# Turning one batch's residual with DMA moves and VectorE transposes, in a Strassen-form MLP kernel

## What is computed

```python
x = decayed_attention(q, k, v, lam)             # laid out as 2 x 768 x 512
h = relu(x^T @ w_tok1) @ w_tok2                 # mixes positions, 768 -> 256 -> 768
u = x + h^T
x = u + relu(u @ w_ch1) @ w_ch2                 # first channel MLP, 512 -> 1536 -> 512
u = x + real(fft2(x))                           # Fourier mixing over positions and channels
un = (u - mean) / sqrt(var + 1e-6)
out = u + relu(un @ w_ch1b) @ w_ch2b            # second channel MLP, 512 -> 2048 -> 512
```

## Time and profile before

| | us |
|---|---|
| median of 3 executions | 566.11 |
| the profiled execution's own time | 565.77 |
| its span, first to last instruction | 563.9 |
| TensorE busy | 559.4 (99%) |
| VectorE busy | 359.0 (64%) |
| GpSimd busy | 256.3 (45%) |
| ScalarE busy | 253.2 (45%) |

### The profile page before, as it was taken

The page is one execution under the profiler, slowest core; times in us unless marked ns, Lnnn a source line. Parts: engine busy times, 40 slices in busy tenths (PEclk is TensorE's granted clock), DMA queues, the critical chain, the costliest instruction groups (busy, mean ns, idle before and its releaser), DMA issues.

```text
span 563.9 us, 9232 instructions
## 1 busy us (share of the span) xinstructions
PE 559.4 (99%) x3412; PEld 499.8 (89%) x3412; DVE 359.0 (64%) x629; ACT 253.2 (45%) x510; POOL 256.3 (45%) x285
## 2 busy tenths in 40 slices
PE   9999999999999999999999999999999999999998
PEld 7889889889989899898988898998989889998996
DVE  5975867766743885467988954679863634344324
ACT  2665335755534444335454443355454433434430
POOL 3663425457534564213767642236563333233301
PEclk9999999999999999999999999999999999999999
DMA  8970303331122121122012220120222212221142
GB/s 324 408 279 3 112 0 118 99 92 52 63 76 74 57 77 60 35 57 74 20 58 75 75 74 20 56 76 20 75 76 75 76 69 63 76 74 57 37 151 112
DMA packets 23726, 48.97 MB, mean 87 GB/s; under 512 B 2170, under 2 KB 3202, under 8 KB 23682
## 3 DMA queue, kind: packets, MB, share of 16 engines
q1 hardware_dynamic: 23088, 46.55, 24.4%
q0 software_dynamic: 448, 1.71, 1.0%
q10 hardware_dynamic: 146, 0.13, 0.1%
HBM read 45.24 MB, written 3.15 MB: 86 GB/s over the span
## 4 chain that ended last, share of the span: by engine, by line
PE 94%; DVE 4%; issue 1%; ACT 0%
PE banks L1200 15%; PE banks L1201 15%; PE banks L1199 15%; PE banks L1479 12%; PE banks L1481 12%; PE banks L1482 12%; PE banks L1272 2%; PE banks L1223 2%; PE banks L1260 2%; PE banks L1316 2%; PE banks L1248 1%; PE banks L1336 1%; PE banks L1211 1%; PE banks L1297 1%; DVE sums L780 1%; PE banks L1229 1%
## 5 line engine op out<-in xcount | busy, mean ns | idle before, releaser
L375 POOL TENSOR_TENSOR w2l<-raw,w2h 128x512 fp32r<-128x512 f32 x56 | 74.2, 1326 | 148.4 <-ACT w2h L513 148.4
L1479 PE MATMUL banks<-th,al 128*128 128x384 f32 x392 | 132.0, 337 | 0.4 <-DVE tl L780 0.2
L1481 PE MATMUL banks<-tl,ah 128*128 128x384 f32 x392 | 132.4, 338 | 0.0
L1482 PE MATMUL banks<-th,ah 128*128 128x384 f32 x392 | 132.1, 337 | 0.0
L513 ACT ACTIVATE snap<-banks 128x384 f32<-128x384 f32 x84 | 41.1, 489 | 126.3 <-PE banks L1482 126.3
L780 DVE TENSOR_TENSOR al<-raw,ah 128x512 fp32r<-128x512 f32 (+1 forms) x112 | 88.5, 810 | 4.9 <-ACT ah L513 3.7
L1077 DVE TENSOR_TENSOR snap<-banks,snap 128x384 f32<-128x384 f32 x84 | 46.5, 553 | 64.9 <-PE banks L1482 64.9
L1479 PEld LDWEIGHTS banks<-th,al 128*128 128x128 f32 x392 | 73.7, 188 | 8.2 <-issue 1.0
L1481 PEld LDWEIGHTS banks<-tl,ah 128*128 128x128 f32 x392 | 73.6, 188 | 6.0
L1482 PEld LDWEIGHTS banks<-th,ah 128*128 128x128 f32 x392 | 73.7, 188 | 0.0
L375 POOL TENSOR_TENSOR raw<-raw 128x256 f32<-128x256 f32 x84 | 69.0, 837 | 2.2
(11 more groups left out here) (182 smaller groups left out, 909.8 us busy)
## 6 DMA issues: line engine op xcount, KB each, us to landing
raw<-w1b_dram SPq DMA_DIRECT2D x16, 512.0 KB, 3.3
raw<-w2b_dram SPq DMA_DIRECT2D x32, 256.0 KB, 2.8
raw<-w1a_dram SPq DMA_DIRECT2D x12, 512.0 KB, 3.3
raw<-w2a_dram SPq DMA_DIRECT2D x24, 256.0 KB, 3.4
kTs<-kT_dram SPq DMA_DIRECT2D x8, 384.0 KB, 9.1
qTs<-qT_dram SPq DMA_DIRECT2D x8, 384.0 KB, 9.7
vns<-vn_dram SPq DMA_DIRECT2D x8, 384.0 KB, 8.8
kns<-kn_dram SPq DMA_DIRECT2D x8, 384.0 KB, 10.1
```

Of the source, the lines that this page charges most:

```text
L375: return nc.gpsimd.tensor_tensor(o, i0, i1, ALU.subtract)
L1479: mm(o[:, 0:HALF], al[:, a, cols], th[b][:, t, k, :], start=start and k == 0, stop=False, skip_group_check=True)
L1481: mm(o[:, 0:HALF], ah[:, a, cols], tl[b][:, t, k, :], start=False, stop=False, skip_group_check=True)
L1482: last = mm(o[:, 0:HALF], ah[:, a, cols], th[b][:, t, k, :], start=False, stop=(k == 1), skip_group_check=True)
```

## The change

Batch 1's residual (`MOVED = 1`) is no longer turned by TensorE. SyncE moves it in 32x32 squares to their transposed places in `th`, where the high parts of T2 to T4 will be written later: 32 DMAs per tile pair, each of four squares (32 partitions x 4 runs of 32 floats). The first 32 stand on SyncE behind a wait for the complete residual and ahead of the loop; those of tile 1 and tile 2 stand behind the down weights of pairs 1 and 2. VectorE then turns each square within itself by four transposes per tile, at the end of pairs 1, 2 and 3 (`turn_squares`), into `tb` and `ts`. The rest of the block work (high parts, sums, low parts) comes one pair later than before, in pairs 2, 3 and 4. ScalarE's copy of B12 goes, and its other two copies read SBUF in place of PSUM. TensorE's side slots are empty in chunk 0, and the counts of `tr_done` are renumbered by `transposed`.

```diff
-SIDE = [{1: BLOCKS[0], 2: BLOCKS[1], 3: BLOCKS[2]},
+SIDE = [{2: BLOCKS[0], 3: BLOCKS[1], 4: BLOCKS[2]},
...
+MOVED = 1
+Q = 32
...
+        def transposed(target, n, half):
+
+            return 2 * event(target - (1 if target > MOVED else 0), n) + half + 1
...
+            def move_squares(n):
+
+                b, t = MOVED % B, TILES[MOVED][n]
+                for i in range(L // Q):
+                    for j in range(L // Q):
+                        rows, to = slice(j * Q, (j + 1) * Q), slice(i * Q, (i + 1) * Q)
+                        for source in range(2):
+                            first = T2 + 2 * source
+                            squares = f(th[b][to, first:first + 2, :, t * L + j * Q:t * L + (j + 1) * Q])
+                            tile = u[rows, NC * b + t + NA * source, :].rearrange("p (k n) -> p k n", k=KD)
+                            sp.dma_start(squares.rearrange("p s k n -> p (s k) n"),
+                                         tile[:, :, i * Q:(i + 1) * Q]).then_inc(s_moved[n], 16)
+
+            sp.wait_ge(u_ready, 2 * NC)
+            move_squares(0)
             for p in range(1, NP):
...
                 down_weights(p, 1)
+                if p < NA:
+                    move_squares(p)
...
             def blocks1_hi(target, n, src):
                 e, b, t = event(target, n), target % B, TILES[target][n]
                 cols = slice(t * L, (t + 1) * L)
-                act.wait_ge(tr_done, 2 * e + 1)
-                if target >= 2:
-                    act.wait_ge(y_added, 4 * (b + 1))
+                if target == MOVED:
+                    act.wait_ge(b1_turned, 2 * n + 1)
+                    copy(th[b][:, B11, :, cols], tb[b][:, B11, :, cols]).then_inc(block_hi, 1)
+                    return
+                act.wait_ge(tr_done, transposed(target, n, 0))
+                act.wait_ge(y_added, 4 * (b + 1))
...
+            def turn_squares(n):
+
+                b, t = MOVED % B, TILES[MOVED][n]
+                cols = slice(t * L, (t + 1) * L)
+                moved = f(th[b][:, T2:T4 + 1, :, cols])
+                dve.wait_ge(s_moved[n], 16 * 2 * (L // Q) ** 2)
+                nc.vector.transpose(tb[b][:, B11, :, cols], moved[:, 0, :, :]).then_inc(b1_turned, 1)
+                nc.vector.transpose(ts[b][:, T3 - T2, :, cols], moved[:, 2, :, :]).then_inc(b1_turned, 1)
+                nc.vector.transpose(tb[b][:, B21, :, cols], moved[:, 1, :, :])
+                nc.vector.transpose(tb[b][:, B22, :, cols], moved[:, 3, :, :]).then_inc(b2_turned, 1)
...
+                if target == MOVED:
+                    b11 = tb[b][:, B11, :, cols]
+                    dve.wait_ge(b1_turned, 2 * n + 2)
+                    minus(ts[b][:, T1 - T2, :, cols], ts[b][:, T3 - T2, :, cols], b11).then_inc(sums_ready, 1)
+                    dve.wait_ge(sums_ready, 2 * e + 1)
+                    dve.wait_ge(block_hi, 2 * e + 1)
+                    minus(tl[b][:, B11, :, cols], b11, f(th[b][:, B11, :, cols])).then_inc(block_lo, 1)
+                    return
...
+                for unit in SIDE[ch].get(j + 1, EMPTY):
+                    if unit and unit[0] == "b1" and ch + 1 == MOVED:
+                        turn_squares(unit[1])
...
-                if units[i] is None:
+                if units[i] is None or ch + 1 == MOVED:
                     return
...
-                units = SIDE[ch].get(j, EMPTY)
+                units = EMPTY if ch + 1 == MOVED else SIDE[ch].get(j, EMPTY)
```

More of the change, by code:

```diff
@@ L193, in build @@
         s_craw = sem("dft_constant_loaded")
+        s_moved = [sem(f"residual_squares_moved_{n}") for n in range(NA)]
+        b1_turned, b2_turned = sem("first_blocks_turned"), sem("second_blocks_turned")
         s_erow, erow_zero = sem("edge_rows_loaded"), sem("edge_rows_zeroed")
@@ L414, in zero_columns @@
                 if b:
-                    pool.wait_ge(tr_done, 2 * event(2, NA))
+                    pool.wait_ge(tr_done, transposed(2, NA - 1, 1))
                     pool.wait_ge(prod_done, 7 * FIRST[2])
@@ L597, in blocks2_hi @@
                 e, b, t = event(target, n), target % B, TILES[target][n]
-                act.wait_ge(tr_done, 2 * e + 2)
+                if target == MOVED:
+                    cols = slice(t * L, (t + 1) * L)
+                    act.wait_ge(b2_turned, n + 1)
+                    copy(th[b][:, B21:B22 + 1, :, cols], tb[b][:, B21:B22 + 1, :, cols]).then_inc(block_hi, 1)
+                    return
+                act.wait_ge(tr_done, transposed(target, n, 1))
                 copy(th[b][:, B21:B22 + 1, :, t * L:(t + 1) * L],
@@ L909, in blocks2_lo @@
                 t2_, t3_, t1_, t4_ = [ts[b][:, k - T2, :, cols] for k in (T2, T3, T1, T4)]
-                b21, b22 = [src[:, i * FH:(i + 1) * FH].rearrange("p (k t) -> p k t", k=2) for i in range(2)]
-                dve.wait_ge(block_hi, 2 * e + 2)
+                if target == MOVED:
+                    b21, b22 = [tb[b][:, k, :, cols] for k in (B21, B22)]
+                    blocks = tb[b][:, B21:B22 + 1, :, cols]
+                    dve.wait_ge(b2_turned, n + 1)
+                else:
+                    b21, b22 = [src[:, i * FH:(i + 1) * FH].rearrange("p (k t) -> p k t", k=2) for i in range(2)]
+                    blocks = src[:, :].rearrange("p (s k t) -> p s k t", s=2, k=2)
+                    dve.wait_ge(block_hi, 2 * e + 2)
                 dve.wait_ge(sums_ready, 2 * e + 1)
@@ L915, in blocks2_lo @@
                 minus(t4_, b21, t2_).then_inc(sums_ready, 1)
-                minus(tl[b][:, B21:B22 + 1, :, cols], src[:, :].rearrange("p (s k t) -> p s k t", s=2, k=2),
-                      f(th[b][:, B21:B22 + 1, :, cols])).then_inc(block_lo, 1)
+                if target == MOVED:
+                    dve.wait_ge(sums_ready, 2 * e + 2)
+                    dve.wait_ge(block_hi, 2 * e + 2)
+                minus(tl[b][:, B21:B22 + 1, :, cols], blocks, f(th[b][:, B21:B22 + 1, :, cols])).then_inc(block_lo, 1)
             def tiles3(x):
@@ L969, in fold_even @@
                     if b:
-                        dve.wait_ge(tr_done, 2 * event(2, NA))
+                        dve.wait_ge(tr_done, transposed(2, NA - 1, 1))
                 if a == 2:
@@ L1046, in ln_norm @@
                 if n == 2:
-                    dve.wait_ge(tr_done, 2 * event(2 + b, 0) + 2)
+                    dve.wait_ge(tr_done, transposed(2 + b, 0, 1))
                 for i in range(2):
```

## The result

The changed kernel takes 602.12 us (median of 4 runs, 601.93 to 603.39) against 565.93 for the kernel before: a ratio of 1.0644, 95% interval [1.0626, 1.0662]. It is 36 us slower. The forecast was 581.5 with a range from 570 to 592: the direction and the place were right, the size was less than half of what happened.

What follows compares the result with a forecast made beforehand. TensorE, busy 99% of the span, was taken to bound the kernel. SyncE's issues delay weight loads, making TensorE 16.3 us late in pair 3; less 0.9 for tile 2's removed groups, +15.4 us, so 581.5, range 570 to 592.

Steps and rivals of the forecast that it cites:

- What bounds the kernel, and the gain: TensorE, busy 99% of the span, bounds; six transpose groups removed from pairs 1 to 3 gain 2.65 us.
- VectorE: Ends of pairs 1 to 3: four square transposes per tile at 0.41 us, 1.6 us per pair, costed at nothing.
- The issue: SyncE's queue: each of 96 moves takes 0.47 us to issue, range from 0.30, upper estimate 0.6.
- c: The time one DMA issue takes on SyncE, set at 0.47 us.
- Pairs 2 and 3: Late weight loads: at most 0.5 us lost in pair 2; A22 of pair 3 makes TensorE 16.3 us late.
- The clock: TensorE's clock may fall behind the stalls; only work after the second counts, 0 to 3 us, costed at nothing.
- The DMA engines: Transfers of the moves: 0.05 to at most 0.76 us per move, taken below the issue time, costed at nothing.
- Rival (b): DMA engines are the bound, at up to 0.76 us per move: +43 us, 609; chance 0.08.
- (c): Faster: SyncE's issues cost next to nothing and the 2.65 us gain is whole, 563.5; chance 0.05.
- (a): Short issue on SyncE, 0.30 to 0.38 us: only pair 1's stall counts, 570 to 573; chance 0.22.

Runs made afterwards that it cites:

- the last one: Against the changed kernel: 16 staged moves in two groups of 8, behind loads of pairs 1 and 2, turning and block work later; 562.93 us, ratio 0.9946.

## Why the prediction was wrong in size

**What bounds the kernel, and the gain.** Right. The removed groups were worth 2.65 us in the forecast, 2.8 in the kernel without moves (563.15 against 565.98) and 3.0 in the last one.

**VectorE.** Right: 0.43 and 0.40 us per transpose against the 0.41 taken from the earlier trace rows, and the kernel without moves shows no wait for them.

**The issue, "I take 0.47".** This is the step that failed. The term was mis-sized: 0.60 us per issue, 0.644 from start to start, 0.66 over a group of 32. Both rows that bounded it have DRAM on one side; the moves have SBUF on both, and that costs 0.2 us more. The number of runs, by which I chose between the two rows, doesn't matter. The form of the sum was right for the loads: its own formulas with c = 0.66 give up_weights(4) landing at 104.4 + 63.4 = 167.8, and GpSimd takes it at 168.06; for up_weights(2) 96.5 + 21.1 = 117.6, against 117.8. As the term enters 96 times, 0.19 us of it are 18 us of the 21 that were missing.

**Pairs 2 and 3.** "At most 0.5 us lost" in pair 2 became 5.6 with the longer issue. The wait that came last in pairs 2 and 3 wasn't the snapshot but down step 6, one position earlier in TensorE's program, 2.8 us behind the landing. I had that price in the chain, but as the release of the next down load alone; the error is half a microsecond, as A22 followed the step at once.

**The clock, "I cost it at nothing".** The granted clock fell to 0.50 in each stop and stayed there for 3.0 to 4.6 us behind it. That only the last stop's share would count was right, and it was 2.2 us, inside the 0 to 3 that stood beside the sum, but not in it. This is nearly all of the 2.4 us that c doesn't explain.

**The DMA engines.** Right for the changed kernel: 13824 more packets added 171 us to the 16 engines' time (24.7% of 16 x 600.3 less 24.4% of 16 x 563.9), 12 ns each, 0.1 us per move against 0.64 for its issue. (Shares of this kind move by themselves: the kernel without moves, with the packets of the kernel before, has 24 us more than it. Counted from there a packet is 11 ns.) Rival (b) is out. The Trainium skill ("DMA: Bandwidth & Descriptors", Why small descriptors are slow (HBM only)) has no penalty for small runs between SBUF and SBUF. The trace agrees in part: a move is far below the 0.76 us that the mean packet would give, but a byte in a run of 128 costs twice what it does in the mean packet of 2 KB (0.10 ns against 0.05). The engines seem to become a limit only where the same runs came in 16 issues, beside the loads.

**The rivals.** (c) stood on the Trainium skill's rule ("DMA: Bandwidth & Descriptors", Issuing engines are not separate DMA queues) that initiating a DMA is usually short beside the DMA itself. For moves of 16 KB the trace shows 0.64 us of SyncE beside 1.8 us from issue to landing, so an issue is a third of its DMA, and far more than the 0.1 us for which each engine is busy. The landings overlap and the issues don't: in a queue of 96 the issues decide. (a) was wrong, though the kernel with half the moves behaves as it would have.

What stays open: why an issue between two SBUF places takes longer. And pair 1 begins at 92.71 to 93.95 us in the profiles of these kernels, though the changes don't touch the program ahead of it (93.11 in the kernel before). The cause is open, and as the gain is 2.7 to 3.0 us, these 1.2 us matter where two variants are compared.

## What to carry to other kernels

A queue that issues DMAs in order is an engine with a program of its own: count issues, not bytes, and ask for each inserted group what stands behind it and when that is due. Price the issue from a row with the same kinds of memory on both sides and a like shape, or measure it, since a term that enters 96 times needs the first care. If an issue's time doesn't depend on its runs, choose a layout in which both sides step evenly, so that one issue carries many pieces, and cut the issues into groups that fit the queue's pauses.

## What was not expected of the hardware

- An issue on SyncE's queue took 0.42 to 0.46 us with DRAM on one side and 0.59 to 0.65 with SBUF on both, from 1 to 24 runs per partition in the latter and for 32 or 128 partitions in either. A single row from DRAM took 0.25.
- Of SBUF-to-SBUF traffic in runs of 128 bytes, 11 to 12 ns of an engine's time per packet; 16 issues of 768 runs each took 11.1 us ahead of the weight loads and 13.7 to 16.1 behind them, a single issue up to 3.5.
- Stops of TensorE of 5.6 us and more were followed by 3 to 6 us of work at half of the full clock (3.0 behind 18.3 us of stop, 5.4 behind 8.9 in the kernel with 16 moves ahead of the loads). Behind the shortest, 3.8 us in the kernel with the moves behind the loads, the clock was still 1.00 when work began and fell within the next microsecond.
